# Keys and queries laid out by dimension, split by GpSimd, with a four-bank score ring

## The reference

```python
q_pool = q.reshape(B, H, S // 2, 2, D).mean(axis=3)
scores = q_pool @ k.transpose(0, 1, 3, 2) / np.sqrt(D)
attn = np.exp(scores - scores.max(-1)); attn /= attn.sum(-1) + 1e-9
x = (attn @ v)                        # to [B * 576, 512]
```

## Time and profile before

| what | value |
|---|---|
| median of three runs | 1389.45 us (1387.18 to 1390.0) |
| the profiled execution | 1389.67 us, span 1387.9 us |
| mean granted TensorE clock | 0.983 of full speed |
| busy over the span: PE, DVE, ACT, POOL | 96%, 38%, 38%, 32% |
| DMA | 103.02 MB, mean 74 GB/s |

### The profile page before, as it was taken

One profiled execution on the slowest core, in us unless ns is written; L12 is line 12 of the kernel. 1 busy time (PEld: TensorE's weight loads), 2 busy tenths in 40 slices (PEclk: granted clock), 3 DMA queues, 4 the chain that ended last, 5 costly groups with the idle time before them and its releaser, 6 DMA issues.

```text
span 1387.9 us, 23084 instructions
## 1 busy us (share of the span) xinstructions
PE 1337.1 (96%) x8036; PEld 1250.5 (90%) x8036; DVE 522.6 (38%) x1350; ACT 528.4 (38%) x1106; POOL 443.1 (32%) x424
## 2 busy tenths in 40 slices
PE   7999999984999999699999999999999999999998
PEld 6999999984999999589899999999999999999998
DVE  6898888872222222324522222122211211221121
ACT  6887878854545554311311312312212212213111
POOL 5333323318757776500400501402302202203200
PEclk9999999996999999899999999999999999999999
DMA  5511111036655665400210200300201201100001
GB/s 148 146 43 36 51 52 51 26 112 212 203 186 168 208 210 173 146 1 1 68 54 1 95 26 0 121 0 30 91 0 35 86 0 60 60 0 0 0 0 68
DMA packets 67994, 103.02 MB, mean 74 GB/s; under 512 B 5471, under 2 KB 24483, under 8 KB 67944
## 3 DMA queue, kind: packets, MB, share of 16 engines
q1 hardware_dynamic: 60008, 86.08, 19.7%
q10 hardware_dynamic: 6464, 11.80, 2.6%
q0 software_dynamic: 1472, 4.54, 1.0%
HBM read 88.42 MB, written 14.16 MB: 74 GB/s over the span
## 4 chain that ended last, share of the span: by engine, by line
PE 93%; DVE 2%; issue 2%; ACT 1%; DMA 1%; POOL 0%; DVEq 0%; SPq 0%; POOLq 0%; ACTq 0%
PE psum L1219 36%; PE psum L1232 28%; PE psum L1251 7%; PE psum L1068 6%; PE psum L1093 5%; PE psum L1078 5%; PE psum L1106 1%; PE psum L1047 1%; PE psum L1264 1%; PE psum L1055 1%; PE psum L1209 1%; ACT acts L517 0%; DMA small<-slots_in 0%; PE psum L1190 0%; ACT wsplit L517 0%
## 5 line engine op out<-in xcount | busy, mean ns | idle before, releaser
L1219 PE MATMUL psum<-acts,wsplit 128*128 128x384 f32 (+1 forms) x3072 | 517.8, 327 | 2.5 <-issue 1.5
L1219 PEld LDWEIGHTS psum<-acts,wsplit 128*128 128x128 f32 x3072 | 508.1, 190 | 5.0 <-issue 1.8
L1232 PE MATMUL psum<-wsplit,acts 128*128 128x512 f32 x1728 | 397.6, 390 | 0.0
L1232 PEld LDWEIGHTS psum<-wsplit,acts 128*128 128x128 f32 x1728 | 323.7, 188 | 66.3
L635 ACT ACTIVATE acts<-psum 128x384 fp32r<-128x384 f32 (+1 forms) x256 | 120.8, 472 | 572.0 <-PE psum L1219 566.4
L437 POOL TENSOR_TENSOR wsplit<-raw,wsplit 128x512 fp32r<-128x512 f32 x128 | 162.6, 1292 | 502.6 <-ACT wsplit L517 502.6
L890 DVE SCALAR_TENSOR_TENSOR acts<-psum,acts 128x384 fp32r<-128x384 f32 (+1 forms) x256 | 136.2, 533 | 375.8 <-ACT acts L635 375.5
L442 POOL TENSOR_TENSOR wsplit<-raw,wsplit 128x512 fp32r<-128x512 f32 x128 | 161.1, 1297 | 134.1 <-ACT wsplit L517 134.1
L517 ACT ACTIVATE wsplit<-raw 128x512 fp32r<-128x512 f32 (+1 forms) x257 | 154.8, 625 | 87.3 <-PE psum L1232 75.2
L1022 DVE SCALAR_TENSOR_TENSOR x<-psum,pr,x 128x512 f32<-128x512 f32 x63 | 47.3, 751 | 293.5 <-PE psum L1232 293.5
L517 ACT ACTIVATE acts<-psum 128x384 fp32r<-128x384 f32 (+2 forms) x282 | 115.3, 458 | 76.3 <-PE psum L1078 44.5
(11 more groups left out here) (123 smaller groups left out, 788.5 us busy)
## 6 DMA issues: line engine op xcount, KB each, us to landing
raw<-in_moe_w_dram SPq DMA_DIRECT2D x64, 1024.0 KB, 5.2
raw<-in_k_dram SPq DMA_DIRECT2D x16, 288.0 KB, 2.9
raw<-in_v_dram SPq DMA_DIRECT2D x16, 288.0 KB, 3.5
slots_in<-zero SPq DMA_DIRECT2D x1, 4608.0 KB
small<-slots_in ACTq DMA_DIRECT2D x8, 576.0 KB, 4.5
small<-in_q_dram SPq DMA_DIRECT2D x16, 256.0 KB, 3.1
slots_out<-small ACTq DMA_DIRECT2D x7, 576.0 KB, 7.1
out_dram<-x ACTq DMA_DIRECT2D x9, 256.0 KB, 2.4
```

What stands on the lines that cost most here:

```text
L1219: last = mm(psum[:, f % HBANKS, 0:w], w1s[a][:, c, f * P:(f + 1) * P], src[z][:, c, cols], start=(i == 0), stop=(i == 3 * DC - 1))
L1232: last = mm(psum[:, bank, :], hs[a][:, f, t0:t0 + P], w2s[z][:, f, :], start=(i == 0), stop=(i == 3 * FC - 1))
```

## The change

The host lays out the keys as [64 dimensions, 1152 positions] for each head, and the queries as [64 dimensions, 2, 576], the two of a pair apart. Each is loaded twice, into partitions 0 to 63 and 64 to 127, with two DMAs of 288 KB. The values are loaded as before, to another place.

- POOL adds the two queries of a pair once, over 128 x 576 (`sum_queries`), rounds the keys over 128 x 1152, and subtracts them in partitions 64 to 127 alone, which leaves hi above lo without a transpose. It also makes hi and lo of the queries. One buffer holds the raw queries of all heads, so the load of the next head's waits for `qs_done`.
- `prep` on PE and `prep_evac` on ACT and DVE are gone. The scale is applied in `move_scores`.
- The scores' ring has four banks, 0, 1, 2 and 7. `turn_out` and `prefix(0)` use banks 1 and 2 of it: the tiles t=0 and t=1 of a head take only banks 2, 7 and 0, in turn.
- At the start ACT issues the loads of head 0's queries; ACT and DVE split head 0's keys in three pieces and its queries. SP issues keys and values of heads 0 and 1, then waits for `qs_done` before the queries of head 1, the gate weights and all else.
- In head 15 `prefix(0)` comes in t=3 ahead of `turn_out(14)`, `place(0)` behind `finish(14)`, and PE doesn't wait for `place`.
- The load of the first expert's w2 half waits only for the keys' last split.

```diff
-        BPT, TBANKS, BPV, BMISC = 3, 3, 6, 7
+        BPT, TBANKS, BPV = 3, 3, 6
+        RING = (0, 1, 2, 7)
+        BTURN, BPOS = RING[1], RING[2]
+        def s_bank(t, c):
+            return RING[(c - 2 if t == 0 else NC * t + c - 1) % 4]
+            def load_keys(g, u):
+                if not (isinstance(g, int) and g < 2):
+                    sp.wait_ge(ks_done, 2 * (g - 2))
+                for a in (0, 1):
+                    sp.dma_start(kraw[u][a * DH:(a + 1) * DH, :], kg[g]).then_inc(k_loaded[u], 16)
+            def load_queries(g):
+                sp.wait_ge(qs_done, g)
+                for a in (0, 1):
+                    sp.dma_start(qraw[a * DH:(a + 1) * DH], qg[g]).then_inc(q_loaded, 16)
+            def load_values(g, u):
+                if not (isinstance(g, int) and g < 2):
+                    sp.wait_ge(vs_done, 2 * (g - 1))
+                sp.dma_start(vraw[u], vg[g]).then_inc(v_loaded[u], 16)
...
-            load_head(0, 0)
-            load_head(1, 1)
+            load_keys(0, 0)
+            load_keys(1, 1)
+            load_values(0, 0)
+            load_values(1, 1)
+            load_queries(1)
             sp.dma_start(wgr[:, :, :], moe2_w_gate.rearrange("(c p) e -> p c e", p=P)).then_inc(wg_loaded, 16)
...
+            def sum_queries(g):
+                pool.wait_ge(q_loaded, 32 * (g + 1))
+                pool.tensor_tensor(qraw[:, 0, :], qraw[:, 0, :], qraw[:, 1, :], ALU.add).then_inc(q_summed, 1)
...
+            sum_queries(0)
             pool.tensor_copy(gfold[:, :, 0:DH], fold[:, :].unsqueeze(1).broadcast_to([P, G, DH])).then_inc(fold_ready, 1)
...
+            def split_head(g, u):
+                pool.wait_ge(k_loaded[u], 32 * loads(g, u))
+                pool.wait_ge(v_loaded[1 - u], 16 * loads(g - 1, 1 - u))
                 if not (isinstance(g, int) and g < 2):
+                    pool.wait_ge(s_ready, SCH * (g - 1))
                 if not (isinstance(g, int) and g < 3):
                     pool.wait_ge(pv_ready, 2 * (g - 2))
+                sum_queries(g)
+                pool.tensor_copy(ksp[u], kraw[u]).then_inc(ks_done, 1)
+                values_hi(g - 1, 1 - u)
+                pool.wait_ge(ks_done, 2 * g - 1)
+                pool.wait_ge(q_summed, g + 1)
+                pool.wait_ge(vs_done, 2 * g - 1)
+                pool.tensor_tensor(ksp[u][DH:P, :], kraw[u][DH:P, :], ksp[u][DH:P, :].bitcast(F32),
                                    ALU.subtract).then_inc(ks_done, 1)
+                pool.wait_ge(ks_done, 2 * g)
+                values_lo(g - 1, 1 - u)
+                pool.tensor_copy(qs[u][0][:, 0:Q], qraw[:, 0, :]).then_inc(qs_hi, 1)
+                pool.wait_ge(qs_hi, g)
+                pool.tensor_tensor(qs[u][1][:, 0:Q], qraw[:, 0, :], qs[u][0][:, 0:Q].bitcast(F32),
+                                   ALU.subtract).then_inc(qs_done, 1)
...
-                    if t < PREP - 1 and not last:
-                        prep_evac(g + 1, 1 - v % 2, t + 1)
-                    if t == QT - 1 and not (last or isinstance(g, int) and g == G - 2):
-                        prep_evac(g + 2, v % 2, 0)
...
-                        1.0, low[:, b, c - 1:c] if c else None, ALU.mult, ALU.min,
+                        QSCALE, low[:, b, c - 1:c] if c else None, ALU.mult, ALU.min,
...
-                    if t == 2 and last:
+                    if t == TURN and not first:
+                        finish(g - 1)
+                    if t == TURN and last:
                         place(0)
-                    if t == 3 and not first:
-                        finish(g - 1)
...
+                if t == 0 and c == 0:
+                    pe.wait_ge(qs_done, g + 1)
+                    if not is_first(g):
+                        pe.wait_ge(ks_done, 2 * g)
+                if t == 2 and c == 0:
+                    if not (isinstance(g, int) and g < 2):
+                        pe.wait_ge(misc_free, g - 1)
+                elif not (is_first(g) and t == 0):
+                    pe.wait_ge(s_moved, SCH * g + NC * t + c - (2 if t == 1 else 3))
...
             def misc(g, v, t):
+                if t == TURN and is_last(g):
+                    pe.wait_ge(s_moved, SCH * G - NC)
+                    prefix(0)
+                if t == TURN and not is_first(g):
+                    turn_out(g - 1)
```

More of the change, by code:

```diff
@@ L104, in build_attention_moe_moe @@
         small = sb("small", [P, 4 * QP + 2 * S + QP])
-        qraw = [small[:, u * QP:(u + 1) * QP].rearrange("p (t c) -> p t c", t=QT) for u in (0, 1)]
-        qdup = [small[:, (2 + u) * QP:(3 + u) * QP].rearrange("p (t a d) -> p t a d", t=QT, a=2) for u in (0, 1)]
+        vraw = [small[:, u * KJ * DH:(u + 1) * KJ * DH] for u in (0, 1)]
+        qraw = small[:, 2 * KJ * DH:2 * KJ * DH + 2 * Q].rearrange("p (two r) -> p two r", two=2)
+        assert 2 * KJ * DH + 2 * Q <= 4 * QP
         rawl = raw[:, 0:2, :].rearrange("p a w -> p (a w)")
@@ L156, in build_attention_moe_moe @@
         consts = sem("consts")
[L157 removed]
+        k_loaded = [sem(f"k_loaded{u}") for u in (0, 1)]
+        q_loaded = sem("q_loaded")
         v_loaded = [sem(f"v_loaded{u}") for u in (0, 1)]
[L159 removed]
+        q_summed = sem("q_summed")
+        qs_hi = sem("qs_hi")
+        qs_done = sem("qs_done")
         vs_done = sem("vs_done")
+        k0_hi = sem("k0_hi")
         k0_done = sem("k0_done")
+        q0_hi = sem("q0_hi")
         ks_done = sem("ks_done")
         misc_ready = sem("misc_ready")
[L164 removed]
         misc_free = sem("misc_free")
@@ L223, in build_attention_moe_moe @@
         DS = 3
[L225 to L228, removed]
+        TURN = 3
         WCH = 2 * FC
         SINK = 8
[L231 to L239, removed]
-        def misc_out(g):
-            if isinstance(g, int) and g >= G - 2:
-                return (PREP + 1) * G - 1 - (G - 1 - g)
-            return (PREP + 1) * (g + 2) - 2 + PREP
-        def misc_after_prep(h):
-            return misc_prep(h, PREP - 1) + 1
+        HBANKS = 4
         def ahead(g, v, t, n):
@@ L1100, in turn_out @@
                 pe.wait_ge(ot_done, 2 * (g + 1))
-                pe.wait_ge(misc_free, misc_out(g))
+                pe.wait_ge(s_moved, SCH * (G if isinstance(g, int) and g >= G - 2 else g + 2))
+                if not is_first(g):
+                    pe.wait_ge(misc_free, g)
                 if is_first(g):
@@ L1165, in _ @@
             pe.wait_ge(consts, 16)
-            for i in range(PREP):
-                prep(0, 0, i)
             for t in (0, 1):
@@ L1356, with _lay @@
 _INS = ["q", "k", "v", "moe_w_gate", "moe_w1", "moe_w2", "moe2_w_gate", "moe2_w1", "moe2_w2"]
+def _lay(inputs):
+    B, H, S, D = inputs["v"].shape
+    laid = dict(inputs)
+    laid["k"] = inputs["k"].reshape(B, H, 128, S // 128, D).transpose(0, 1, 4, 3, 2).reshape(B, H, D, S)
+    laid["q"] = inputs["q"].reshape(B, H, S // 2, 2, D).transpose(0, 1, 4, 3, 2)
+    return laid
 def kernel(**inputs):
```

199 lines of the change are left out of this document (57 added, 142 removed).

## The result

| | before | after |
|---|---|---|
| median of the runs, us | 1388.5 to 1389.7 by job | 1380.11 (1379.36 to 1381.87, 4 runs) |
| profiled execution, us (span) | 1389.67 (1387.9) | 1380.57 (1378.8) |

The ratio is 0.994 (95% interval 0.9925 to 0.9954): 0.6% faster, 9.4 us of the 17.3 that I forecast. The direction and the range of 1366 to 1382 held; the forecast of 1372.2 was 8 us off, so nearly half of the forecast gain is missing. That 1380.11 lies in the range is luck: the range had been widened for two rivals of which neither happened, and the forecast's own reach was 1367 to 1377.

A forecast was written before the change was run, and what follows sets the result against it. PE bounds a head at 18.0 us, DVE close behind, and ACT's loop holds t=2. Terms 17.1 + 0.8 - 1.8 - 3.0 + 4.3 = 17.4 us off 1389.67 gave 1372.3, median 1372.2; 8-in-10 range 1366 to 1382.

The forecast's parts named there:

- two rivals: ACT's loop doesn't bind (1367, chance 0.08) and DVE becomes the limit (1381, chance 0.12); range 1366 to 1382 includes both.
- What is removed in a head: Attention heads: transposes go, ACT's loop holds t=2; 1.25 us a head, 17.1 us over 14 heads.
- The rival in which ACT's loop doesn't bind: Tile t=2: output copy moves up, all 1.63 us come off each head, 5.3 us more, 1367; chance 0.08.
- What comes back: DVE's two stops where the loop over four heads goes back: shorter tiles lose cover, 1.8 us lost.
- The end: Head 15: DVE's subtractions no longer behind `place`, last 18 value products begin 4.3 us sooner; lower bound 3.2.
- The scores' ring: Scores' banks in the heads: the new ring costs nothing that the forecast could find.
- The start: First score move waits behind `qs_done` and the gate load, 15.8 us; 3.0 us lost, bounds 0.9 to 4.6.
- POOL: Splitting queries and keys: 9.8 us a head, loop with load 13.6 against 16.6, covered by PE, cost 0.
- the rival in which POOL is the bound: POOL's 9.8+3.75 loop turns out longer than a head; with 20 us heads grow, 1417; chance 0.10.
- Head 0: Head 0, already at the loop's pace: 0.8 us gained in its last two tiles.
- The rest moves up unchanged: Behind the end of attention: everything only comes earlier, with no gain or loss of its own.
- DVE becomes the limit: Heads: 15.8 us of DVE work in 16.6, misfits take half the heads' gain, 1381; chance 0.12.

The follow-up runs named there:

- the moved products: Changed kernel with three value products per head moved from tile t=3 to t=2: 1376.87 us, ratio 0.9912.
- the one with four edits: Changed kernel with gate load early, three value products in t=2, row sums' reduction without 1e-9, experts' early subtractions behind batch 1's scatter: 1369.46 us, ratio 0.9856.
- the late lower parts: Changed kernel with GpSimd's first two weight subtractions of expert 0 moved behind the scatter of batch 1: 1380.45 us, ratio 0.9942.

## Why the prediction was off

- **What is removed in a head** (1.25 us, and PE back to 16.6 with ACT holding t=2): right. Undisturbed heads fell from 17.92 to 16.65, by 1.27 where I had 1.25, and the chain goes through ACT at the end of t=2. The rival in which ACT's loop doesn't bind is refuted by that chain and by the 0.4 a head that the moved products found idle there.
- **What comes back** (DVE's stops, 1.8): right, 1.75.
- **The end** (4.3): right in size and in the path through DVE's `place`, 4.73 for what lies behind `turn_out` of head 13. The doubt went the other way: I had lowered the bound to 3.2 in case PE ran at half its clock after the change, but the low clock (0.53 to 0.56) stood behind PE's wait for `place` in the kernel before, and in the change, without that wait, it was 1.00.
- **The scores' ring** (nothing): right in the heads, by the run with three banks.
- **The start** (3.0, bounds 0.9 to 4.6): the step that failed most; it cost 6.5, outside its bounds. PE's first product came at 12.07, too, 0.4 later than its first scores before, where I had said no later. The order of the path was right, but I let it begin with the queries, at the time they land. The keys, landing at 8.65, and their halves on ACT and DVE stand ahead of the queries' subtraction in the engines' own order, 2 us; dearer issues, load and subtraction are another 1.2, most of the last a wait for POOL, and 0.3 was rounded off in the forecast. The gate load moved up takes back 6.0 to 6.5 us.
- **POOL** (9.8 us a head, a loop of 13.6, cost 0): the size was right (9.65 from the start of the sum at 68.53 to the end of the last subtraction at 78.18, and a loop of 14.6), and the rival in which POOL is the bound fell; it begins to bind where the loop, 14.6 now, passes 16.65, and the run with 3.6 us more in it is beyond that point. But "by that rule the term stays 0, since `p_lo` and `move_scores` read PSUM" was incomplete: I went through the large instructions and left out the row sums, and the two small subtractions with both inputs in SBUF, 128x32 at the start and 128x80 behind attention. The Trainium skill (SBUF — State Buffer, Who interferes with whom) names `tensor_scalar` without an accumulator among the DVE instructions that can enter a mode in which they use the port pair shared with GpSimd, so that the two can lock each other out; its sentence on instructions with at most one SBUF input holds only outside such modes, a condition that my prediction dropped. The runs agree: 0.17 us became up to 2.57, and the reduction stayed at 0.15 beside the same POOL instruction. In the change it cost 0.9 us in head 3, and in head 1 the instruction was 0.5 longer (0.69); what PE paid for that isn't shown.
- **Head 0** (+0.8): missed, it gained nothing. From the first turn to `turn_out` of head 0 the forecast had 1.65 us of gain (0.8, and 0.85 in t=0 and t=1 of head 1), and it became 0.3 of loss. The nine matmuls of the first turn took 2.18 us where they took 1.20 before, and their weight loads 1.78 where they took 0.96, though the records show a granted clock of 1.00 for both. I took it for a PE that comes from idle time. Two runs speak against that, the one with the gate load alone and the one with four edits. In both PE began 4.5 us before its first turn and worked for nearly all of that time, and yet the loads are slow in one and fast in the other:

```profile
16.30 1.59 PEld L1036 LDWEIGHTS psum<-ident,small 128*128 128x128 f32 x9 [0.80 <-ACT small L524]
16.91 0.96 PEld L1034 LDWEIGHTS psum<-ident,small 128*128 128x128 f32 x9 [0.88 <-ACT small L522]
```

  The stretch took 28.1 and 28.3 us in the two runs with the early gate load and slow loads, and 27.4 to 27.8 in the four with fast ones. So a slow first turn costs some 0.7 us, and why it is slow stays open.
- **"The rest moves up unchanged"**: wrong by 1.9. The moved stretch met POOL's work in full (2.32 us for a subtraction that takes 0.24 alone and took 0.41 before); shown by the late lower parts, though the median didn't follow.
- **DVE becomes the limit** had the nearest time, 1381, and the wrong cause: heads are at 16.65, not halfway back.

The remaining 0.6 us is in the experts, within what that part varies from one execution to the next. The sum itself has a slip of 0.1: 1372.3 less 0.2 is 1372.1.

## What to carry to other kernels

When a start is costed, write down what stands ahead in each engine's own order, not only the transfer that the last wait names: here SP, ACT and DVE each had the keys in front. When work moves to GpSimd, go through every DVE instruction that it will lie beside, the five-column ones too, and ask for its form. The reserve of an engine is the length of its loop, load included, against the period, and not its idle share; and a stretch that moves earlier should be looked at for what it now meets: one gain here uncovered a queue stop that had always been there. And a gain of 2 us in a total should be looked for in the dates: a row sum that meets POOL in one execution and not in the next, or a lower clock behind a stop, is as large.

## What the runs showed of the hardware

- A `tensor_scalar` of 128x5 on DVE, SBUF to SBUF, took 0.17 us alone and up to 2.57 beside GpSimd (with three additions inside the loop), up to the end of GpSimd's running instruction; a `tensor_reduce` of the same data took at most 0.16.
- A `tensor_tensor` on DVE with both inputs in SBUF: 128x32 took 0.19 us alone, 0.81 and 1.16 beside a `tensor_tensor` of GpSimd; 128x80 took 0.24 alone, 0.41 and 2.32 beside two.
- At each place where the loop over four heads goes back DVE stood for 2.4 to 3.0 us in the kernels before and after; the granted clock behind such a stop was 1.00 in some executions and 0.63 to 0.74 in others.
- GpSimd: a subtraction of 64 partitions x 1152 took 2.65 us, 128 x 576 took 1.43: the columns count, not the partitions. A rounding of 1152 columns took 1.14 against 0.66 for 576, less than twice; I had used twice for both.
- A transfer of 4.6 MB held the next issue on the same queue for 14.8 to 15.0 us; one of half the size held it for 7.5.
- Head 0's key load (two transfers of 288 KB, with the other first loads beside it) took 7.17 us to land, where a query load of the same size took 4.3 in the median.
